# A three-stage attention, soft-MoE and MLP kernel on one core: another order at the MLP's head, its last two blocks taken tile by tile, and four unused products behind the first up product

## The reference

```
attention, per batch and head:  scores = q k^T / 8 - slope_h * |i - j|, only for 0 <= i - j < 128; softmax; times v
x = heads side by side                        # 2304 x 512
soft MoE:  logits = x phi                     # 2304 x 32 (8 experts x 4 slots)
           slots  = softmax_over_tokens(logits)^T x            # 32 x 512
           slot_out[e] = relu(slots[e] w1[e]) w2[e]            # 512 -> 1024 -> 512
           c = softmax_over_slots(logits); x2 = c slot_out     # 2304 x 512
MLP:       h = x2 w_in (512 -> 2048);  g = max(0.01 h, h);  out = g w_out (2048 -> 512)
```

## Time and profile before

| what | value |
|---|---|
| median of 3 runs | 390.22 us (389.74 to 390.31) |
| profiled execution: its own time | 390.76 us |
| its span in the trace | 389.0 us |
| PE busy | 376.5 us (97%) |
| PE weight loads busy | 288.0 us (74%) |
| DVE busy | 220.4 us (57%) |
| ACT busy | 195.0 us (50%) |
| POOL busy | 12.5 us (3%) |

### The profile page before, as it was taken

One profiled execution on the slowest core, in us unless ns is written; L12 is line 12 of the kernel. 1 busy time (PEld: TensorE's weight loads), 2 busy tenths in 40 slices (PEclk: granted clock), 3 DMA queues, 4 the chain that ended last, 5 costly groups with the idle time before them and its releaser, 6 DMA issues.

```text
span 389.0 us, 9358 instructions
## 1 busy us (share of the span) xinstructions
PE 376.5 (97%) x3515; PEld 288.0 (74%) x3515; DVE 220.4 (57%) x763; ACT 195.0 (50%) x527; POOL 12.5 (3%) x46
## 2 busy tenths in 40 slices
PE   5999999999999999789999999999999999999996
PEld 3788877867785333467888888888888888888885
DVE  6776576665574273397866444644464464445443
ACT  5888878778762012476644334334334434433431
POOL 1200000000000100021100000000000000000000
PEclk9999999999999999999999999999999999999999
DMA  7798789769999999980000100200020002002002
GB/s 250 274 335 303 258 277 318 260 243 348 396 383 386 386 386 386 385 304 4 3 0 35 48 0 1 83 0 0 2 82 0 3 0 81 2 0 82 2 1 81
DMA packets 27214, 62.09 MB, mean 160 GB/s; under 512 B 2081, under 2 KB 2593, under 8 KB 27169
## 3 DMA queue, kind: packets, MB, share of 16 engines
q1 hardware_dynamic: 27024, 61.33, 43.8%
q10 hardware_dynamic: 144, 0.16, 0.1%
HBM read 56.77 MB, written 4.72 MB: 158 GB/s over the span
## 4 chain that ended last, share of the span: by engine, by line
PE 89%; DMA 5%; DVE 3%; SPq 1%; ACT 1%; issue 1%; POOL 0%; DVEq 0%; ACTq 0%; POOLq 0%
PE bank L862 10%; PE bank L864 10%; PE bank L863 10%; PE turned L557 6%; PE bank L590 6%; PE bank L533 6%; PE turned L863 6%; PE turned L864 6%; PE turned L862 5%; PE bank L579 5%; PE bank L847 4%; PE bank L763 4%; DMA slot<-in_moe_w_out_dram 3%; PE turned L607 3%; PE bank L873 1%; DMA qk<-in_k_dram 1%
## 5 line engine op out<-in xcount | busy, mean ns | idle before, releaser
L1457 DVE SCALAR_TENSOR_TENSOR g_sb<-bank,h_sb 128x384 f32<-128x384 f32 x93 | 51.8, 557 | 93.6 <-ACT h_sb L1133 93.4
L1133 ACT COPY h_sb<-bank 128x384 f32<-128x384 f32 x93 | 44.5, 478 | 118.9 <-PE bank L847 118.6
L864 PE MATMUL bank<-w_hi,g_lo 128*128 128x512 f32 x180 | 70.9, 394 | 0.0
L862 PE MATMUL bank<-w_hi,g_hi 128*128 128x512 f32 x180 | 70.6, 392 | 0.1
L863 PE MATMUL bank<-w_lo,g_hi 128*128 128x512 f32 x180 | 70.7, 393 | 0.0
L959 ACT ACTIVATE prob<-prob,row_min 128x192 f32<-128x192 f32 (+1 forms) x144 | 51.9, 440 | 3.9 <-DVE row_min L1211 3.9
L1464 DVE TENSOR_TENSOR g_lo<-g_sb,g_hi 128x384 fp32r<-128x384 f32 x93 | 51.0, 549 | 0.1
L1138 ACT CAST g_hi<-g_sb 128x384 fp32r<-128x384 f32 x93 | 48.0, 516 | 0.2 <-DVE g_sb L1457 0.2
L967 ACT COPY probT<-turned 128x384 f32<-128x384 f32 (+1 forms) x76 | 33.4, 443 | 20.2 <-PE turned L557 19.1
L533 PE MATMUL bank<-qk 64*64 64x192 f32 (+2 forms) x576 | 35.8, 325 | 5.1 <-DMA qk<-in_q_dram 4.0
L862 PEld LDWEIGHTS bank<-w_hi,g_hi 128*128 128x128 f32 x180 | 33.8, 188 | 9.1 <-DVE g_lo L1464 1.7
(11 more groups left out here) (169 smaller groups left out, 435.2 us busy)
## 6 DMA issues: line engine op xcount, KB each, us to landing
slot<-in_moe_w_dram SPq DMA_DIRECT2D x22, 1024.0 KB, 8.5
slot<-in_moe_w_dram SPq DMA_DIRECT2D x5, 2048.0 KB, 16.0
v<-in_v_dram SPq DMA_DIRECT2D x16, 325.0 KB, 4.5
qk<-in_q_dram SPq DMA_DIRECT2D x15, 288.0 KB, 4.6
qk<-in_k_dram SPq DMA_DIRECT2D x15, 288.0 KB, 5.3
slot<-in_moe_w_in_dram SPq DMA_DIRECT2D x4, 1024.0 KB, 14.3
slot<-in_moe_w_out_dram SPq DMA_DIRECT2D x8, 512.0 KB, 11.7
out_dram<-o_sb SPq DMA_DIRECT2D x5, 768.0 KB, 3.6
```

Of the source, the lines that this page charges most:

```text
L862: nc.tensor.matmul(acc, hi, w_hi[:, f, :], start=(f == 0), stop=False)
L864: last = nc.tensor.matmul(acc, lo, w_hi[:, f, :], start=False, stop=(f == FT - 1))
L1133: nc.scalar.copy(h_sb[:, f % 2, :], bank[6 + f % 2][:, 0:GW]).then_inc(h_copied, 1)
L1457: nc.vector.scalar_tensor_tensor(out=g_sb[:, f % 2, :], in0=bank[6 + f % 2][:, 0:GW], scalar=0.01, in1=h_sb[:, f % 2, :], op0=ALU.mult, op ...
```

## The change

Three things are changed.

At the MLP's head, PE does `project(0)` first, then `combine_T(3)`, then `project(1)`. ACT rounds the slices of g ahead of the first slice of w_out: `split_g(0)`, `split_g(1)`, `split_w_first(0)`, `split_g(2)`, `split_g(3)`, and only then the copies of `up`'s first result. `split_w_first(1)` moves behind the copy of h for slice 1. DVE has its `split_w_first(0)` behind `split_g(2)`, and `split_g(3)`, `split_g(4)` each one place earlier.

Behind `up(0,0,0)` PE issues four products of 128x512 into bank 1. Nothing reads them; the bank is later started afresh.

At the end, the last two slices (14 and 15) of the last group are taken tile by tile: six products for tile 0, six for tile 1, six for tile 2, instead of slice by slice. DVE copies tile 2 in two halves of 256 columns; SP stores the left half, and ACT's queue the right half. The number of stores goes from 8 to 9.

```diff
@@ sync: the last stores
-                sp.dma_start(out[row0:row0 + P, :], o_sb[:, t, :]).then_inc(out_stored, 16)
-            sp.wait_ge(out_stored, 16 * (NG - 1 + GT))
+                cols = slice(0, DM // 2 if t == GT - 1 else DM)
+                sp.dma_start(out[row0:row0 + P, cols], o_sb[:, t, cols]).then_inc(out_stored, 16)
+            sp.wait_ge(out_stored, 16 * (NG + GT))
@@ tensor
+            def keep_busy(n):
+                for i in range(n):
+                    nc.tensor.matmul(bank[1][:, :], c_stack[:, TAIL:TAIL + P], c_stack[:, TAIL:S], start=True, stop=True)
...
-            pe.wait_ge(c_hi_done, 3)
-            pe.wait_ge(c_lo_done, 3)
-            combine_T(3, C_BANK[3])
...
             project(0)
+            pe.wait_ge(c_hi_done, 3)
+            pe.wait_ge(c_lo_done, 3)
+            combine_T(3, C_BANK[3])
             project(1)
@@ tensor, first_block
                 up(0, 0, 0)
+                keep_busy(4)
                 pe.wait_ge(w_hi_done, 1)
@@ tensor, the end of the last group
+            def last_blocks(par):
+                for t in range(GT):
+                    for f in (FT - 2, FT - 1):
+                        if t == 0:
+                            pe.wait_ge(glo_done, (NG - 1) * FT + f + 1)
+                        for kind in range(3):
+                            g, w = ((g_hi, w_hi), (g_hi, w_lo), (g_lo, w_hi))[kind]
+                            last = nc.tensor.matmul(bank[GT * par + t][:, :], g[:, f % NR2, t * P:(t + 1) * P], w[:, f, :],
+                                                    start=False, stop=(f == FT - 1 and kind == 2))
+                    last.then_inc(acc_done, 1)
...
-                        down(grp, par, FT - 2)
-                        down(grp, par, FT - 1)
+                        last_blocks(par)
@@ scalar
-            split_w_first(0)
...
                 split_g(0)
                 split_g(1)
-                split_w_first(1)
+                split_w_first(0)
+                split_g(2)
+                split_g(3)
                 act.wait_ge(h_done, 1)
...
-                split_g(2)
+                split_g(4)
                 copy_h(1)
-                split_g(3)
+                split_w_first(1)
                 round_g(1)
                 copy_h(2)
                 split_w(1)
                 round_g(2)
-                split_g(4)
                 split_g(5)
...
+            act.wait_ge(acc_copied, GT * NG + 1)
+            act.dma_start(out[NG * GW - P:NG * GW, DM // 2:DM], o_sb[:, GT - 1, DM // 2:DM]).then_inc(out_stored, 16)
@@ vector, copy_acc
-                    nc.vector.tensor_copy(o_sb[:, t, :], bank[GT * par + t][:, :]).then_inc(acc_copied, 1)
+                    parts = 2 if known(grp) and grp == NG - 1 and t == GT - 1 else 1
+                    for i in range(parts):
+                        cols = slice(i * DM // parts, (i + 1) * DM // parts)
+                        nc.vector.tensor_copy(o_sb[:, t, cols], bank[GT * par + t][:, cols]).then_inc(acc_copied, 1)
```

## The result

| | kernel before | changed kernel |
|---|---|---|
| median | 391.62 us (389.74 to 394.72, 12 runs) | 389.28 us (387.71 to 393.85, 12 runs) |
| ratio to before | | 0.9940 (95%: 0.9917 to 0.9964) |
| profiled execution: time, span | 390.76, 389.0 us | 389.20, 387.4 us |
| PE busy | 376.5 us | 378.6 us |

The change gains 0.60%, 2.3 us of the 391.6. The forecast was 2.3 us less, too; but it was pinned to a median of 390.22, which three runs had given, and the measured 389.28 lies above the range of 387.0 to 389.0.

A forecast was written before the change was run, and what follows sets the result against it. PE's chain of waits was taken as the bound, with removable gaps in the MLP's head. Head 2.3 us less, last two slices 0, halves +0.0: 390.22 - 2.3 = 387.9 us, 8-in-10 range 387.0 to 389.0.

The forecast's parts named there:

- The number: Whole kernel: median forecast as 390.22 less 2.3 us, which is 387.9 us.
- `up` of slice 0: MLP's head: starts at 162.44 instead of 163.26 us, 0.8 us earlier, with PE's own work the late part.
- Slice 3 and POOL: MLP's head: `up` of slice 3 at 166.6 instead of 168.95 us, 2.3 us earlier, the wait for POOL gone.
- Slice 6: MLP's head: `up` of slice 6 at 174.8 instead of 177.57 us, 2.7 us earlier.
- The new wait at `down` of slice 5: MLP's head: PE waits 0.4 us for DVE's `lower_g(5)`, leaving a gain of 2.3 us.
- The four products: Behind the first `up`: they last until 163.58 us, cover 0.4 us wide, cost nothing.
- The end: Last two slices and halved last tile: 0 for PE, and +0.0 us for the halves, between -0.2 and +0.2.
- the landing of 128 KB: Last tile's half store: slope gives 1.7 us, other end 2.1; taken as 2.1 less about 0.15.
- The two half copies: DVE's last tile: 0.43 us per half, right half done 0.17 us later than the whole was.
- B: Head: DVE and ACT become the bound already at slices 1 to 3; gain 0.8 to 1.6 us, 389.0 us; chance 0.20.
- C: DVE faster than its rows, no wait at `down(5)`, half lands in 1.7 us: 2.7 + 0.2, 387.3 us; chance 0.10.
- D: PE's clock falls to 1.2 GHz once the head's product pattern changes, so slower: 10 us give 392.9 us; chance 0.03.

The follow-up runs named there:

- e10: Changed kernel with `project(1)` replacing the four unused products and ACT's `split_g(3)` behind slice 0's rounded pieces, run again: ratio 0.9937 to the kernel before, median 388.42 us.
- e9: The changed kernel run once more, unaltered: ratio 0.9932 to the kernel before, median 389.51 us.
- e11: The kernel before with only the four unused products added behind the first `up`: ratio 1.0002 to the kernel before, median 391.83 us.
- e5: Changed kernel with DVE's old list put back: `up` of slice 3 at 9.14 us and slice 6 at 17.76 us behind the anchor.
- e2: The kernel before with only the new end (last two slices tile by tile, halves on two queues): ratio 1.0007 to the kernel before.
- e1: Changed kernel with the last two slices, whole copy and stores of before put back: ratio 0.9958 to the kernel before.
- e4: Changed kernel with eight unused products instead of four: ratio 0.9962 to the kernel before; slice 6 at 16.42 us behind the anchor.
- e3: Changed kernel without the four unused products: ratio 0.9978 to the kernel before; slice 6 at 16.15 us behind the anchor.
- e6: Changed kernel with the four transposes ahead of `project(0)` again: `up` of slice 0 at 3.78 us and slice 6 at 16.57 us behind the anchor.
- e7: Changed kernel with the last tile copied whole and stored by SP in one piece: last product's start to span's end 3.60 us.
- e12: Changed kernel without the four unused products, run again: ratio 0.9938 to the kernel before, median 389.36 us.

## Why the prediction was right in its steps and wrong in its number

**The number.** The step that failed is the last of the sum: "the forecast for the median is 390.22 - 2.3". The change moved the time by 391.62 - 389.28 = 2.3 us, as forecast, but the base was 1.4 us too low, and the range held no term for that. It came from three runs that lay within 0.6 us of each other; the next nine runs of the same kernel gave 391.1 to 394.7. Of the 76 runs of it beside the experiments only 12 were at 390.31 or less. Whether the three were chance or the level itself moves from one series of runs to another is open. The profiles show where the spread arises. The anchor, ahead of which all these kernels have the same work in the same order, lies between 158.64 (e10) and 164.59 us (e9): 6 us of spread before the change's first instruction. Behind it there is little: slice 6 of the changed kernel's head lies at 16.13 to 16.16 in all its profiles, and from the anchor to the end of the span the changed kernel takes 227.9 and 227.4 us (e9), the old head with the old end 229.8 and 229.5 (e11). Why the attention's length varies so I didn't study, beyond e9's pause.

That 2.3 us came out to the tenth is in part luck. The forecast had it all in the head, which gave less (2.07, and 1.85 against an old head without the late load), while the end gave 0.25, which had been put at nothing.

**`up` of slice 0**, predicted 0.8 us earlier, was 0.47. The new order was right and PE's own list is what it waits for, but that list is 0.35 us longer than I had made it. `project(0)` starts 1.00 us behind the anchor and not 0.88; it now comes right behind the copies of `soT` that it needs, and I take that to be the reason, though no bracket shows it. And a run of `project` takes 1.01 us, not 0.90, when products of 128 columns of weights follow it (160.53 to 161.54, and 162.13 to 163.14), where 0.90 was its time in front of another run like it.

**Slice 3 and POOL**: right in kind. Predicted 2.3 us earlier, measured 1.94 from the anchor; the missing 0.4 is the term above. POOL's copy, taken at 0.61, needed 0.29. e5 shows the mechanism: put DVE's order back and 1.32 us of wait for POOL returns. The small waits that were forecast next came, too: from `up` of slice 3 to its trio PE takes 167.82 - 167.36 = 0.46 us, where 0.18 is the time without a wait.

**Slice 6**: predicted 2.7, measured 2.23. **The new wait at `down` of slice 5**: predicted 0.4, and it is there with 0.17 on PE, smaller since PE came later. So slice 8 is 2.07 earlier against a forecast of 2.3. Against an old head without the late load (group 1's slice 0 at 42.1 in e2 and e11, 40.24 in e1) the head gives 1.85.

**The four products**: right, no cost; their cover is 0.35 us wide, and e4 put the price of leaving it where the sum had it.

**The end**: I took 0 and it was -0.24 to -0.28. The term that was mis-sized most is the landing of 128 KB: I stayed near the 2.1 us of 256 KB, and the straight line through 256 and 768 KB, 1.7, was right. The two half copies were over-sized as well, 0.43 us each where they took 0.38: the last copy ends 385.22 - 384.04 = 1.18 us behind the last product's start, and it was 386.48 - 385.36 = 1.12, so they cost 0.06 and not 0.17. The Trainium skill's fixed 2 us ("DMA: Bandwidth & Descriptors", section "Anatomy of one DMA"), by which the halves would have been a loss, isn't borne out: the measured 1.7 to 1.8 lies under it. That section is on DMAs that GpSimd starts, and these are SP's and ACT's.

**The rivals**: B didn't come about: PE loses at most 0.3 us at a place in slices 1 to 3; C was half right, in the end's term. For D I had written that the rows grant 1.00 in the half-idle head; one profile had not been enough for that: in four of ten executions of the old head the mean clock was lower, and the one drop placed lay in the head. It still gave no term. Head and end together: 1.85 to 2.07 plus 0.25, which is 2.1 to 2.3 us, less what PE's pace takes in some executions (0.3), and the runs gave 2.3 with an interval of 1.4 to 3.3, which holds all of these.

## What to carry to other kernels

Where PE waits for a small chain over two or three engines, write the engines' lists side by side with measured start-to-start times and move what nobody waits for yet behind what somebody does: DVE's new order, in which two operations of 0.3 us move ahead of two and three others and one of 0.7 us moves back, was worth 1.6 us. Fill a wait with work that must be done anyway rather than with unused work. And forecast the change, not the level: three runs close together say little about the median of the next ten, so a range needs a term for the base, and positions should be compared from a point just ahead of the change.

## What the runs showed of the hardware that I had not expected

In e2 TensorE's granted clock fell to 0.50 in the old head, where PE's waits had been 0.38 and 1.31 us; in the profile of before the waits there were 0.68 and 1.31, and the clock stayed at 1.00. So one profile doesn't tell what the clock does in other executions: 37 of 86 with the old head had a lower mean.

POOL's copy of 64x128 took 0.29 us for slice 3 of the changed kernel, and 0.61 in the kernel before. Each time that it took 0.61 to 0.74 us in the heads of these two profiles, DVE was at work beside it on a remainder of w or g with both inputs in SBUF (`w_lo` or `lower_g`). That this is what slows it down was not tested; but a forecast that takes the copy from one row can be off by 0.3 us.

PE's pace changes slightly at a granted clock of 1.00. A slice takes 2.24 us in the kernel before and in most stretches of all profiles, but in the changed kernel's profile it takes 2.25 in others, above all from the middle of group 4 on, and the difference adds up to 0.3 us. Two `up` of the last group, first in the changed kernel, then before:

```profile
366.66 0.34 PE L853 MATMUL bank<-c_stack,g_stack 128*128 128x384 f32 x1
368.91 0.34 PE L853 MATMUL bank<-c_stack,g_stack 128*128 128x384 f32 x1
```

```profile
368.07 0.34 PE L847 MATMUL bank<-c_stack,g_stack 128*128 128x384 f32 x1
370.31 0.34 PE L847 MATMUL bank<-c_stack,g_stack 128*128 128x384 f32 x1
```

e3, e5, e6 and e7 show such stretches too, e1, e9, e10 and e12 hardly any. e9 is the same kernel as the first, so it isn't the change. What it comes from is open.
